# Reordering one matrix product by its contraction tile, and moving a weight load and three copies, in a fused attention and MLP kernel on one core

## The reference

```
scores = (q @ k^T) / 8, masked to 0 <= pos_q - pos_k < 64; attn = softmax(scores)
x      = attn @ v                                  # heads side by side: [B, 576, 512]
h      = relu(x @ w_in)                            # [B, 576, 1024]
c      = 3-tap convolution of h along the sequence, one set of taps per column
x2     = (h * sigmoid(c)) @ w_out                  # the "down" product, contraction over 1024
u, v   = halves of relu(x2 @ w_in2); v normalised over its columns
out    = (u * (w_spatial @ v + b_spatial)) @ w_out2
```

## Time and profile before

| | |
|---|---|
| median of 3 runs | 527.55 us (527.09 to 529.13) |
| profiled execution, its own time | 525.97 us |
| its span, first to last instruction | 524.2 us |
| PE busy | 498.7 us, 95% of the span |
| PEld busy | 466.1 us, 89% |
| DVE busy | 268.0 us, 51% |
| ACT busy | 252.6 us, 48% |
| POOL busy | 70.4 us, 13% |
| mean granted TensorE clock | 0.993 |

### The profile page before, as it was taken

How to read it: one execution, slowest core, us unless ns; L and a number is a source line. 1 busy time by engine, 2 the same in 40 slices (tenths; PEclk the granted TensorE clock), 3 DMA queues, 4 the chain that set the end, 5 groups by cost and what they waited for, 6 DMA issues and landing times.

```text
span 524.2 us, 10566 instructions
## 1 busy us (share of the span) xinstructions
PE 498.7 (95%) x4432; PEld 466.1 (89%) x4432; DVE 268.0 (51%) x543; ACT 252.6 (48%) x646; POOL 70.4 (13%) x91
## 2 busy tenths in 40 slices
PE   4888999999989999999999999999999999999997
PEld 3678988899978999888999988988999899989997
DVE  3865956638846469556389226635034502541040
ACT  4857855438645277454488156326112622262111
POOL 4693003300023100033000021001000200020000
PEclk9979999999999999999999999999999999999999
DMA  8791001350002610014800100000100020002002
GB/s 269 249 365 45 0 1 38 93 235 2 1 2 81 236 48 0 1 43 122 275 1 1 40 2 2 0 1 23 68 1 1 1 91 1 2 0 91 1 0 91
DMA packets 15587, 33.10 MB, mean 63 GB/s; under 512 B 1330, under 2 KB 4402, under 8 KB 14772
## 3 DMA queue, kind: packets, MB, share of 16 engines
q1 hardware_dynamic: 13284, 28.22, 15.6%
q10 hardware_dynamic: 2256, 4.21, 2.3%
HBM read 27.71 MB, written 4.72 MB: 62 GB/s over the span
## 4 chain that ended last, share of the span: by engine, by line
PE 87%; ACT 4%; DMA 3%; DVE 3%; issue 2%; POOL 1%; SPq 0%; ACTq 0%; DVEq 0%
PE dense L354 63%; PE dense L539 11%; PE x_ps L401 4%; PE pt_ps L388 3%; ACT vp L594 3%; PE score L375 3%; PE score L369 2%; DMA vp<-w_out 1%; DVE negmax L773 1%; DMA vp<-v_rows 1%; DMA qk<-q_t 1%; POOL vrstd L1044 0%; DVE qk L903 0%; DVE wr L878 0%; DVE bias L777 0%
## 5 line engine op out<-in xcount | busy, mean ns | idle before, releaser
L354 PE MATMUL dense<-ar,wr 128*128 128x288 f32 x1152 | 163.2, 298 | 2.8 <-issue 2.8
L354 PE MATMUL dense<-xr,wr 128*128 128x288 f32 x1152 | 156.9, 297 | 2.6 <-ACT tmp L620 2.2
L354 PEld LDWEIGHTS dense<-ar,wr 128*128 128x128 f32 x1152 | 154.5, 188 | 5.3 <-issue 3.9
L354 PEld LDWEIGHTS dense<-xr,wr 128*128 128x128 f32 x1152 | 154.5, 189 | 3.6 <-ACT tmp L620 2.4
L822 DVE SCALAR_TENSOR_TENSOR tmp<-tmp,taps 128x576 f32<-128x576 f32 x64 | 53.5, 837 | 28.7 <-ACT tmp L626 27.4
L1007 POOL TENSOR_TENSOR vp<-vp,recip 128x512 f32<-128x512 f32 x36 | 37.4, 1040 | 183.2 <-DVE recip L798 183.2
L539 PE MATMUL dense<-wr,ar 128*128 128x288 f32 x448 | 60.2, 295 | 0.0
L539 PEld LDWEIGHTS dense<-wr,ar 128*128 128x128 f32 x448 | 59.7, 188 | 0.0
L594 ACT ACTIVATE vp<-score,bias 128x128 f32<-128x128 f32 x128 | 45.3, 366 | 27.1 <-DVE bias L777 26.8
L354 PE MATMUL dense<-wr,xr 128*128 128x512 f32 (+1 forms) x240 | 55.3, 390 | 0.0
L354 PEld LDWEIGHTS dense<-wr,xr 128*128 128x128 f32 (+1 forms) x240 | 42.3, 177 | 11.6
(11 more groups left out here) (75 smaller groups left out, 463.2 us busy)
## 6 DMA issues: line engine op xcount, KB each, us to landing
vp<-v_rows SPq DMA_DIRECT2D x36, 256.0 KB, 2.9
out_t<-vp SPq DMA_DIRECT2D x16, 288.0 KB, 2.1
qk<-k_t SPq DMA_DIRECT2D x3, 1152.0 KB, 7.4
qk<-q_t SPq DMA_DIRECT2D x3, 1152.0 KB, 9.3
x2keep<-w_in ACTq DMA_DIRECT2D x2, 1024.0 KB, 6.6
qk<-w_in SPq DMA_DIRECT2D x1, 2048.0 KB, 8.1
x2keep<-w_out ACTq DMA_DIRECT2D x1, 1280.0 KB, 7.3
vp<-w_spatial_t SPq DMA_DIRECT2D x1, 1152.0 KB
```

The costliest lines, as they stand in the source:

```text
L354: last = mm(dst, stationary(a, t), moving(c, t), start=(t == 0 and n == 0), stop=(t == (of or len(tiles)) - 1 and n == 2))
```

## The change

- The down product's pieces are ordered by contraction tile: for t = 0 to 5 the four accumulators (d 0 and 1, c 0 and 1) each take tile t, then each of the four takes tiles 6 and 7. Output tiles 2 and 3 follow as before. The last batch uses the same order. TensorE waits for each gated tile as it comes to it, where it waited for five (four in the last batch), then seven, then eight.
- The shares become 28, 4, 4, 4, 4, 4, 3, 3, 3, 3, 2, 2.
- `raw_out_b` lies where the convolution's buffers `conv` will be. It is issued in step 6, ahead of `raw_out_a`, and its tiles 5, 6, 7 are split first. The first taps of `up(0)` wait for their low parts (`split_lo_early`).
- SP issues q and k of batch 1 only once `raw_out_a` has landed.
- `keep_x2` moves from the end of the step in which its tile is finished to the end of the next step's VectorE work.
- ScalarE no longer waits for all of w_out's low parts after `up(0)`.

```diff
-        raw_out_b = carve(vp, 3 * D, FT - OUT_A, D)
+        raw_out_b = carve(tmp, 3 * (S + 2), FT - OUT_A, D)
...
+        OUT_ORDER = [*range(OUT_A, FT), *range(OUT_A)]
...
-        def down_pieces(early):
-            pieces = [(d, c, t) for d in range(2) for c in range(2) for t in range(early)]
-            pieces += [(0, c, t) for ts in (range(early, FT - 1), range(FT - 1, FT)) for c in range(2) for t in ts]
-            pieces += [(1, c, t) for c in range(2) for t in range(early, FT)]
+        def down_pieces():
+            pieces = [(d, c, t) for t in range(FT - 2) for d in range(2) for c in range(2)]
+            pieces += [(d, c, t) for d in range(2) for c in range(2) for t in range(FT - 2, FT)]
             return pieces + [(d, c, t) for d in range(2, KT) for c in range(2) for t in range(FT)]
...
-        SHARES = [24, 4, 4, 4, 4, 4, 4, 4, 3, 3, 3, 3]
+        SHARES = [28, 4, 4, 4, 4, 4, 3, 3, 3, 3, 2, 2]
...
                 sp.wait_ge(score_done, NB * b + NB)
+                if b == 0:
+                    sp.wait_ge(out_loaded[0], 16)
...
                 if n == 0:
-                    pe.wait_ge(split_lo_out, N_PIECES)
-                    pe.wait_ge(gated_lo, FT * b + early)
+                    pe.wait_ge(split_lo_early, OUT_FIRST)
+                    pe.wait_ge(split_lo_out, N_PIECES - OUT_FIRST)
...
-                if d == 0 and c == 0 and t in (early, FT - 1):
-                    pe.wait_ge(gated_lo, FT * b + (FT - 1 if t == early else FT))
+                if d == 0 and c == 0:
+                    pe.wait_ge(gated_lo, FT * b + t + 1)
...
+                        if n < OUT_FIRST:
+                            act.wait_ge(split_lo_early, min(n + 2, OUT_FIRST))
                         nc.scalar.activation(conv[:, f % 4, :], h_pad[:, f % 3, 0:S], ACT.Copy,
...
                 elif t == 6:
+                    act.dma_start(raw_out_b, w_out_t[:, OUT_A:FT, :]).then_inc(out_loaded[1], 16)
                     act.dma_start(raw_out_a, w_out_t[:, 0:OUT_A, :]).then_inc(out_loaded[0], 16)
...
-                if t == STEPS - 2:
-                    act.wait_ge(trans_done, NB)
-                    act.dma_start(raw_out_b, w_out_t[:, OUT_A:FT, :]).then_inc(out_loaded[1], 16)
-                for i in {STEPS - 3: (0, 1), STEPS - 2: (2, 3), STEPS - 1: (4, 5, 6, 7)}.get(t, ()):
+                for i in {STEPS - 3: OUT_ORDER[0:2], STEPS - 2: OUT_ORDER[2:4], STEPS - 1: OUT_ORDER[4:]}.get(t, ()):
...
-            act.wait_ge(split_lo_out, N_PIECES)
...
             def attention_step(t, b):
...
                     copy_transposed(t - 2, start + t - 2, start)
+                if t and b:
+                    for d in WHOLE.get(t - 1, ()):
+                        keep_x2(d, b - 1)
...
                     attention_step(t, b + 1)
-                    for d in WHOLE.get(t, ()):
-                        keep_x2(d, b)
```

More of the change, by code:

```diff
@@ L167, in program @@
         split_lo_out = sem("split_lo_out")
+        split_lo_early = sem("split_lo_early")
         in2_hi = sem("in2_hi")
@@ L249, in score_view @@
             return t[:, :, 0:2 * P]
-        def down_pieces(early):
-            pieces = [(d, c, t) for d in range(2) for c in range(2) for t in range(early)]
-            pieces += [(0, c, t) for ts in (range(early, FT - 1), range(FT - 1, FT)) for c in range(2) for t in ts]
-            pieces += [(1, c, t) for c in range(2) for t in range(early, FT)]
+        def down_pieces():
+            pieces = [(d, c, t) for t in range(FT - 2) for d in range(2) for c in range(2)]
+            pieces += [(d, c, t) for d in range(2) for c in range(2) for t in range(FT - 2, FT)]
             return pieces + [(d, c, t) for d in range(2, KT) for c in range(2) for t in range(FT)]
-        EARLY = FT - 3
-        PIECES = down_pieces(EARLY)
-        SHARES = [24, 4, 4, 4, 4, 4, 4, 4, 3, 3, 3, 3]
+        PIECES = down_pieces()
+        SHARES = [28, 4, 4, 4, 4, 4, 3, 3, 3, 3, 2, 2]
         ENDS = [sum(SHARES[:i + 1]) for i in range(len(SHARES))]
@@ L444, in up, with down_piece @@
                     last.then_inc(h_filled, 1)
-            def down_piece(n, b, pieces, early, drained, drained_at):
-                d, c, t = pieces[n]
+            def down_piece(n, b, drained, drained_at):
+                d, c, t = PIECES[n]
                 if n == 0:
-                    pe.wait_ge(split_lo_out, N_PIECES)
-                    pe.wait_ge(gated_lo, FT * b + early)
[L453 to L458, removed]
-                if d == 0 and c == 0 and t in (early, FT - 1):
-                    pe.wait_ge(gated_lo, FT * b + (FT - 1 if t == early else FT))
+                    pe.wait_ge(split_lo_early, OUT_FIRST)
+                    pe.wait_ge(split_lo_out, N_PIECES - OUT_FIRST)
+                if t == 0 and c == 0:
+                    if d < 2:
+                        pe.wait_ge(relu_done, FT * b + FT - 1 + d)
+                    else:
+                        pe.wait_ge(drained, drained_at + d - 1)
+                if d == 0 and c == 0:
+                    pe.wait_ge(gated_lo, FT * b + t + 1)
                 last = product(dense[d % 2][:, c, 0:HALF], lambda a, t: wout[a][:, t, d * P:(d + 1) * P],
@@ L484, in _ @@
                         for n in range(ENDS[t] - SHARES[t], ENDS[t]):
-                            down_piece(n, b, PIECES, EARLY, x2_kept, KT * b + 1)
+                            down_piece(n, b, x2_kept, KT * b + 1)
                 pe.wait_ge(x2_kept, KT * b + KT)
                 up(b + 1)
-            last_pieces = down_pieces(FT - 4)
-            for n in range(len(last_pieces)):
-                down_piece(n, B - 1, last_pieces, FT - 4, x2_lo, 0)
+            for n in range(len(PIECES)):
+                down_piece(n, B - 1, x2_lo, 0)
             def v_part(m, tiles):
@@ L851, in _ @@
                     dve.wait_ge(split_hi_out, i + 1)
-                    vec.tensor_tensor(wout[1][:, i, :], raw_out(i), wout[0][:, i, :].bitcast(F32),
-                                      ALU.subtract).then_inc(split_lo_out, 1)
+                    o = OUT_ORDER[i]
+                    vec.tensor_tensor(wout[1][:, o, :], raw_out(o), wout[0][:, o, :].bitcast(F32),
+                                      ALU.subtract).then_inc(split_lo_early, 1)
             dve.wait_ge(zero_cols, 1)
@@ L1021, in _ @@
                 pool.wait_ge(split_hi_out, i + 1)
-                pl.tensor_tensor(wout[1][:, i, :], raw_out(i), wout[0][:, i, :].bitcast(F32),
+                o = OUT_ORDER[i]
+                pl.tensor_tensor(wout[1][:, o, :], raw_out(o), wout[0][:, o, :].bitcast(F32),
                                  ALU.subtract).then_inc(split_lo_out, 1)
```

## The result

The changed kernel takes 521.93 us, median of 4 runs (521.27 to 522.66), against 527.66 us for the kernel before in the same comparison (527.09 to 529.13): a ratio of 0.9888, 95% interval 0.9861 to 0.9914. That is 5.7 us faster, where 2.0 were forecast (525.5, range 523.2 to 528.5). The profiled execution took 521.27 us, its span 519.5 against 524.2.

A forecast was written before the change was run, and what follows sets the result against it. TensorE, busy for 95% of the span, was taken as the bound, so only waits were summed: -1.6 - 0.7 + 0.3 = -2.0 us. The new median was forecast at 525.5 us, range 523.2 to 528.5.

The forecast's parts named there:

- Part 1: Start to `up(0)`: w_out's last tiles sooner remove the 2.16 us relu wait, less 0.6 us lost: -1.6 us.
- The second term: Before block 6's values: v rows landing late cost 1.1 us, partly repaid when the clock returns: +0.6 us.
- Rival C: Start: low clock stretch from 29.5 to 36.3 shortens or vanishes, up to 3.4 us, to 522.1; chance 0.10.
- 768 KB more put it 1.93 us later: Block 6's v rows, served behind the larger w_out load, land at 31.1 instead of 29.2.
- rival B: Block 6's v rows are not late, so the 0.6 us is not lost: 524.8 us; chance 0.22.
- Part 2: Before the first share of pieces: order by contraction tile removes the 0.92 us stall in each attention batch.
- Part 3: Attention steps under the new shares: -0.2 to -0.3 us a batch, -0.7 us for three batches.
- Part 4: VectorE's moved copies to `x2keep`: zero either way; if exposed, 0.76 us a batch.
- Part 5: Last batch's down product: piece 2 waits for its relu, piece 32 perhaps for a split; together +0.3 us.
- rival F: Down product: changing PSUM banks every three matmuls costs clock, 52 us, to 577; chance 0.02.
- D: Start: longer idle before block 6's values keeps the clock low to 43.1, giving 529.4 us; chance 0.10.
- E: `up(0)`: late splits or slowed convolution keep the 2.16 us relu wait, 527 to 528 us; chance 0.09.

The follow-up runs named there:

- e1: Kernel before with only the w_out loads, their splits and SP's wait changed, old order and shares: 522.86 us against 528.08.
- e5: Kernel before with only ScalarE's splits of w_out's tiles 5 to 7 moved into `up(0)`, loads unchanged: 524.84 us against 527.53.
- e10: Kernel before with SP holding q and k of batch 1 until `raw_out_b` has landed: 523.01 us against 528.42.
- e3: Kernel before with twelve filler matmuls in TensorE's idle time of batch 0's attention: 528.12 us against 528.08.
- e2: Kernel before with only the new piece order, shares and place of the x2 copies, old w_out loads: 528.01 us against 528.08.
- e6: Kernel before with splits late in `up(0)`, new order, shares and copies, last batch in old order: 522.19 us against 527.53.
- e9: Kernel before with eight filler matmuls where TensorE waits in `up(0)` for the first relu: 525.79 us against 528.42.
- e4: The changed kernel run again without an edit: 521.53 us against 528.08 for the kernel before.
- e7: Changed kernel with the last batch's pieces in their old order: 520.82 us against 527.53 for the kernel before.
- e8: Changed kernel without SP's wait ahead of q and k of batch 1: 522.29 us against 527.53 for the kernel before.
- e11: Changed kernel with last batch in old order and the taps' load issued by SP at the start: 521.61 us against 528.42 before.
- e12: Changed kernel with twelve filler matmuls after steps 8 and 9 of batch 0's attention: 521.61 us against 528.42 before.

## Why the prediction was wrong

**Part 1 failed, in both terms of its sum, "-2.16 + 0.6 = -1.6 us".** The mechanism of the first was right: ScalarE's first relu stood behind the landing of raw_out_b, and with the load sooner TensorE does not wait (e1), nor when only the split is moved (e5), and it waits 0.23 us when the landing alone is made earlier (e10). Its size was wrong, by taking the wait of one profiled execution for what its cause costs: with the clock kept up the same landing costs a wait of 4.59 us and 1.5 us of slow matmuls behind it (e3). The second term, +0.6 for late v rows under a low clock of unchanged length, did not come at all. Three things were missed.

First, TensorE's restart in `up(0)` was set by the landing, 44.23 to 45.03 us in the three profiles with before's loads, with nothing added to the wait (before, e2, e3), whenever TensorE got there. The low-clock stretch from 29.5 to 36.3 us lay ahead of a wait, so it cost nothing; it only shortened the wait, which is 4.59 us with the clock kept up (e3). Once the landing no longer sets the restart, the clock counts. The forecast added the low stretch of before to the changed kernel as if its cost were in both. Rival C had the right stretch with the wrong account: it priced the clock's return at 3.4 us, where the changed kernel's executions at mean clocks of 0.993 and 1.00 are 1.4 us apart (522.66 and 521.27). Between the two profiles, the 4.5 us are the wait of 2.16, 2.07 by which the 36 matmuls ahead of it start sooner (34.95 against 37.02), and 0.3 that I do not account for. The 2.07 come from the absent low stretch, and that is at least in part luck of the execution: the stretch was 6.8, 6.8, 0, 3.4, 3.4 and 6.8 us long with before's loads (before, e2, e5, e6, e9, e10) and 0, 3.4, 0, 6.8, 0 and 0 with the new ones (the changed kernel, e1, e4, e7, e8, e11). Whether the new loads also make it rarer, so few profiles don't tell. In e1 it was half as long and cost about 1 us (59.95 against 59.00). The changed kernel's own execution at a mean clock of 0.993, which is that of before's profile, took 522.66 us, 3.3 less than before's 525.97.

Second, the wait itself brought a second low-clock stretch behind it, 3.4 us long and 1.5 us dear (e2, e3; gone in e9 with fillers). The one profile of before happened not to have it. That this execution took 525.97 us, less than any of its three runs (527.09 to 529.13), was in the table; the forecast scaled by 0.3% where it should have asked what the usual execution has more. That the 1.6 to 2 us are mostly this is my reading of e9, not measured by itself.

Summed by the profiles: in e3, whose total is that of before, the scores of batch 1 begin at 65.61; in the changed kernel at 59.00. Of these 6.6 us, 4.6 are the wait, 1.5 the second stretch and 0.2 the earlier start of the 36 matmuls (34.95 against 35.16); 0.3 I do not account for. This agrees with e4's 6.5 us between medians.

Third, **the v rows** were not made late by the change. In its profile they landed 7.6 us after their issue, at 30.6, and TensorE started block 6's values at 30.63, 0.5 us later than in the profile of before. But this is spread between executions. The same load took 6.3, 7.3, 7.6, 7.1, 7.1, 7.6 and 6.2 us with 1280 KB issued ahead of it (before, e2, e3, e5, e6, e9, e10), and 7.6, 6.2, 7.5, 6.2, 6.2, 7.5 and 6.7 with 2048 KB (the changed kernel, e1, e4, e7, e8, e11, e12). So the step "768 KB more put it 1.93 us later" failed, and rival B was right on this term. The rows are of the changed kernel's load and e1's:

```profile
vp<-v_rows SPq DMA_DIRECT2D x1, 256.0 KB, 7.6
```
```profile
vp<-v_rows SPq DMA_DIRECT2D x1, 256.0 KB, 6.2
```

The 97.3% of the earlier trace rows was read as "served behind". The changed kernel's queues show more, first from 24 to 27 us and then from 27 to 28:

```profile
q10 hardware_dynamic: 495, 0.98, 87.6%
```
```profile
q10 hardware_dynamic: 111, 0.23, 58.3%
q1 hardware_dynamic: 82, 0.17, 43.0%
```

From 24 to 27 us SP's queue (q1) moved no packet in either kernel; from 27 us on both queues moved some at once, and raw_out_a, issued before the v rows, landed 2.5 us after them, at 33.1. The Trainium skill (DMA: Bandwidth & Descriptors, Queues, rings and completion order) has the engines take turns between queues. The rows from 27 us on agree with that; why SP's load moved nothing in the 4 us behind its issue, no row tells.

One cost was not in the sum: the taps' load is now third in ScalarE's queue. Its issue took 0.55 us in three profiles and 1.74, 1.84 and 2.79 in three others (e8, e12, e7), where TensorE stood 1.9 to 3.0 us before the values of block 4; behind 1280 KB alone it took 0.55 to 0.82. (A slip without effect: 44.23 less 2.16 is 42.07 and not 42.05.)

**Part 2 was right.** The 0.92 us before the first pieces are gone. e5 and e6 show that the order is worth more when VectorE is late, 2.81 us, and in e1 1.08 us.

**Part 3 was right.** The first share ends at 71.04, 11.3 us behind the scores; the two new waits on exponentials are 0.24 us each where 0.33 was forecast, since TensorE's own steps took a little more; the last step takes 103.95 - 102.28 = 1.67 us, as worked out. Three batches: -0.6 against -0.7.

**Part 4**: nothing shows, as forecast. It was not tried by itself.

**Part 5 was right in sign and low in size**: +0.54 us against +0.3. Putting back the old order gave 25.44 us again (e11). Both causes that the forecast named are there. Read one by one in the trace, the matmuls start 0.133 us apart but for two places: from 273.22 to 273.76 two steps take 0.54 us, 0.28 more than they should, where piece 2 waits for its relu (+0.2 forecast), and from 285.47 to 285.95 two take 0.48, 0.21 more, where piece 32 waits for the first split, which ends at 284.89 + 0.76 = 285.65 (0 to 0.2 forecast). The alternation of PSUM banks costs nothing: the first share's 84 matmuls take 11.37 us, 0.135 each, as before, and the clock is 1.00 (rival F).

Rival B's v rows came, but they are a small part of the difference; D and E did not come. The sum failed in part 1 alone: -4.5 us between the profiles where -1.6 stood, and a further 1 us between the medians.

## What to carry to other kernels

A wait in a profile is what is left after everything ahead of it; what its cause holds back is found by asking when the releaser comes, and what would run ahead of it otherwise. Before sizing a stall from one profiled execution, compare that execution with the median: if it is the fastest, something in the usual one is missing from the rows. And look at what shares the DMA engines with a late transfer, in other queues too: here 2304 KB that nobody wanted for 30 us went ahead of 768 KB that held up the whole kernel, and one wait (e10) brought 5.4 us, where versions of the changed kernel brought 6.8 in the same comparison (e11, e12).

## What the runs showed of the hardware

- TensorE's clock fell to its lower level not only in the thin start but again behind a wait: at 45.2 us behind one of 3.16 us (e2), at 44.9 behind one of 4.59 (e3), and at 62.3 near the end of one of 2.81 (e5). In e2 and e3 the matmuls had restarted by then. It stayed low for 3.4 us each time. Behind before's wait of 2.16 us it did not fall. Filling the wait with useless matmuls made the kernel faster (e9).
- The early low-clock stretch was 0, 3.4 or 6.8 us long in executions that run the same instructions up to it (e5, e6, before).
- The issue of a 12 KB DMA took 0.55 to 2.79 us when it was the third in ScalarE's queue behind 2048 KB, and ScalarE's instructions stood behind it (e7); as the second behind 1280 KB it took 0.55 to 0.82. The two loads ahead of it took 0.38 and 0.51 us to issue.
- A v load of 256 KB issued 0.4 us behind raw_out_a's 1280 KB in another queue landed 2.5 us before it, 7.6 us after its issue; the median of the 36 such loads in the profile of before is 2.9 us. With 1280 or 2048 KB issued ahead of it, it took 6.2 to 7.6 us alike.
- 768 KB in ScalarE's queue took 7.1 us to land while q, k and v rows in SP's queue had 85.4% of the engines' time, and 4.5 us with those held back (e10).
